# Logits of the second routing: from turned results instead of extra columns of w2

## What is computed

```python
x = attention(r, k, v, w, u)                       # [3072, 384]
# first mixture: top 1
logits = x @ w_gate + modality_bias[modality_id]
e_idx, gate = argmax(logits), softmax(logits)[e_idx]
for e in range(8):
    y[mask] = gate[mask] * (relu(x[mask] @ w1[e]) @ w2[e])
# second mixture: top 2 with noise
logits = y @ w_gate2
noise_scale = log1p(exp(y @ w_noise))
noisy = logits + noise_scale * noise
top2, weights = two largest of noisy, softmax over the two
out[mask] += weight * (relu(y[mask] @ w1b[e]) @ w2b[e])
```

## Time and profile before

| | us |
|---|---|
| three runs | 985.29, 985.99, 988.22 |
| median | 985.99 |
| the profiled execution | 981.03 |
| its span in the trace | 979.2 |

### The profile page before, as it was taken

One profiled execution on the slowest core, in us unless ns is written; L12 is line 12 of the kernel. 1 busy time (PEld: TensorE's weight loads), 2 busy tenths in 40 slices (PEclk: granted clock), 3 DMA queues, 4 the chain that ended last, 5 costly groups with the idle time before them and its releaser, 6 DMA issues.

```text
span 979.2 us, 22988 instructions
## 1 busy us (share of the span) xinstructions
PE 918.4 (94%) x7093; PEld 882.1 (90%) x7094; DVE 554.1 (57%) x1247; ACT 258.5 (26%) x493; POOL 423.3 (43%) x460
## 2 busy tenths in 40 slices
PE   5999999899889989999689999999999999999995
PEld 4888888899889989988689999999999999999995
DVE  8888989667754545648583544425335344443532
ACT  2222333124322323424220222203122231321210
POOL 7333333424655554446553343433434434344232
PEclk9999998989989999989899999999999999999998
DMA  8787899305411111123424534425333444513223
GB/s 266 229 263 256 268 353 359 111 3 188 169 34 51 33 34 41 42 98 93 139 66 90 131 96 115 111 44 117 104 52 101 121 104 112 112 32 54 45 48 51
DMA packets 61848, 115.96 MB, mean 118 GB/s; under 512 B 14352, under 2 KB 42192, under 8 KB 61776
## 3 DMA queue, kind: packets, MB, share of 16 engines
q1 hardware_dynamic: 39552, 75.37, 23.1%
q0 software_dynamic: 18336, 34.91, 17.2%
q10 hardware_dynamic: 3888, 4.80, 1.4%
HBM read 83.63 MB, written 31.51 MB: 118 GB/s over the span
## 4 chain that ended last, share of the span: by engine, by line
PE 78%; DVE 10%; issue 5%; POOL 2%; DMA 2%; DVEq 1%; ACT 1%; another core or an unknown queue 0%; ACTq 0%; SPq 0%; POOLq 0%
PE ps L1894 21%; PE ps L1895 20%; PE ps L1896 20%; PE ps L1841 3%; PE ps L1796 2%; PE ps L1800 2%; PE ps L1765 2%; PE ps L1742 2%; PE ps L1827 2%; PE ps L1854 1%; PE ps L1790 1%; DVE grow L1042 1%; PE ps L1750 1%; DVE hid_lo L1557 1%; DVEq L388 1%
## 5 line engine op out<-in xcount | busy, mean ns | idle before, releaser
L1894 PE MATMUL ps<-x_hi,weights 128*128 128x256 f32 x984 | 282.2, 287 | 18.9 <-issue 12.3
L1895 PE MATMUL ps<-x_lo,weights 128*128 128x256 f32 x984 | 281.2, 286 | 2.1 <-issue 2.0
L1896 PE MATMUL ps<-x_hi,weights 128*128 128x256 f32 x984 | 280.6, 285 | 2.5 <-issue 2.4
L1894 PE MATMUL ps<-weights,hid_hi 128*128 (+1 forms) x616 | 220.0, 357 | 3.4 <-DVE hid_lo L1557 2.3
L1895 PE MATMUL ps<-weights,hid_hi 128*128 (+1 forms) x616 | 212.5, 345 | 0.8 <-issue 0.8
L1896 PE MATMUL ps<-weights,hid_lo 128*128 (+1 forms) x616 | 211.5, 343 | 0.0
L1894 PEld LDWEIGHTS ps<-x_hi,weights 128*128 128x128 f32 x984 | 189.0, 192 | 21.0 <-issue 20.5
L929 ACT ACTIVATE hid_hi<-ps 128x512 fp32r<-128x512 f32 x164 | 97.1, 596 | 411.9 <-PE ps L1896 373.5
L1557 DVE SCALAR_TENSOR_TENSOR hid_lo<-ps,hid_hi 128x512 fp32r<-128x512 f32 x164 | 112.1, 690 | 153.2 <-ACT hid_hi L929 130.1
L1895 PEld LDWEIGHTS ps<-x_lo,weights 128*128 128x128 f32 x984 | 189.1, 192 | 6.3 <-issue 6.2
L1896 PEld LDWEIGHTS ps<-x_hi,weights 128*128 128x128 f32 x984 | 189.0, 192 | 2.9 <-issue 2.9
(11 more groups left out here) (313 smaller groups left out, 1148.8 us busy)
## 6 DMA issues: line engine op xcount, KB each, us to landing
stage<-in_w_dram SPq DMA_DIRECT2D x18, 1536.0 KB
kv_in<-in_kv_T_dram SPq DMA_DIRECT2D x24, 512.0 KB, 5.8
kv_in<-in_kv_T_dram SPq DMA_DIRECT2D x24, 448.0 KB, 4.0
w_in<-in_w_T_dram SPq DMA_DIRECT2D x24, 258.5 KB, 4.6
moe_rows<-zeros SPq DMA_DIRECT2D x26, 192.0 KB, 4.0
out_dram<-zeros SPq DMA_DIRECT2D x26, 192.0 KB
x_rows<-y_tok ACTq DMA_DIRECT2D x24, 192.0 KB
w2T_raw<-in_w_T_dram SPq DMA_DIRECT2D x2, 1536.0 KB
```

Source lines behind the costliest of these rows:

```text
L1894: pe.matmul(out_ps, hi, by_hi, start=first, stop=False)
L1895: pe.matmul(out_ps, hi, by_lo, start=False, stop=False)
L1896: return pe.matmul(out_ps, lo, by_hi, start=False, stop=final)
```

## The change

The 16 extra columns go. `CW` becomes 384, and `expert_columns`, `split_v`, `low_v`, `load_w2T` and the table `v_now` are removed with the transposed copy of w2. Instead, for every row, PE transposes the copied results (`turn_results`: six transposes of `sy`), ACT copies them out of PSUM (`turned_copies`, two), PE multiplies them with the 16 columns (`result_logits`: six products) and ACT copies the logits (`logits_copy`). The places in a step move: `turn_results` after `up` quarter 0, `result_logits` after quarter 1, `row_logits` after `hidden_low` 1, `row_first` after 2, `row_second` after 3, `row_ranks` just ahead of the last 12 products of `down`, and `row_places` behind both tiles of `split_x`. `turn_results` waits for `s_rankread`, which DVE raises in `row_places` when it has read the ranks of the row before, and for `s_oc[0]`, ACT's copy of the results. In step 0 of `l = 1`, `split_x` of both tiles now stands ahead of `second_order`.

```diff
-    CW = C + 2 * E
+    CW = C
...
+            def turned_copies(n, banks):
+                for t in range(TS):
+                    act.wait_ge(s_turn, n * TS + t + 1)
+                    act.nop(nofuse=True)
+                    act.activation(turned[t][:, :, :], banks[t], ACT.Copy).then_inc(s_turnc, 1)
+
+            def logits_copy(n, k):
+                act.wait_ge(s_logits, n)
+                act.nop(nofuse=True)
+                act.activation(raw_all[:, k, :, :], logit_ps, ACT.Copy).then_inc(s_raw, 1)
...
-                        act.activation(raw_all[:, u, t, :], o_ps[t][:, C:CW], ACT.Copy).then_inc(s_raw, 1)
-                        act.activation(sy[u][:, t, :], o_ps[t][:, 0:C], ACT.Copy).then_inc(s_oc[0], 1)
+                        act.activation(sy[u][:, t, :], o_ps[t], ACT.Copy).then_inc(s_oc[0], 1)
...
                 then(dve.tensor_tensor(row_pos[:, :, :], rank_ps, filled[:, 1:3, :], ALU.add))
+                dve.sem_inc(s_rankread, 1)
...
                     if peeled and s == 0:
                         hidden_low(0, 0)
+                        row_logits(last, raw_all[:, 0, :, :], last_nz, 2, last_dst)
+                        hidden_low(0, 1)
                         row_first(last, last_nz)
+                        hidden_low(0, 2)
                         row_second(last)
-                        hidden_low(0, 1)
-                        row_places(last, last_nz, 2, last_src, None)
-                        hidden_low(0, 2)
                         hidden_low(0, 3)
                         split_x(1, 1, 0)
+                        row_places(last, last_nz, 2, last_src, None)
+                        split_x(1, 1, 1)
                         second_order()
-                        split_x(1, 1, 1)
...
-                def expert_columns(n, v):
-                    pe.wait_ge(s_wT, n * 16 + 16)
-                    for m in range(FC):
+                def turn_results(n, rows, banks):
+                    pe.wait_ge(s_oc[0], 1 + n * TS)
+                    pe.nop(nofuse=True)
+                    for t in range(TS):
                         for c in range(CC):
-                            last = pe.matmul(v[:, m, :], w2T_raw[:, c, m * P:(m + 1) * P], gate_w[1][:, c, :],
+                            last = pe.transpose(banks[t][:, c, :], rows[:, t, c * P:(c + 1) * P], ident[:, :])
+                        last.then_inc(s_turn, 1)
+
+                def result_logits(n):
+                    pe.wait_ge(s_turnc, n * TS)
+                    pe.nop(nofuse=True)
+                    for t in range(TS):
+                        for c in range(CC):
+                            last = pe.matmul(logit_ps[:, t, :], turned[t][:, c, :], gate_w[1][:, c, :],
                                              start=(c == 0), stop=(c == CC - 1))
-                        last.then_inc(s_vmm, 1)
+                    last.then_inc(s_logits, 1)
...
                     up(s, 0, run)
+                    if l == 0 and (not peeled or s >= 2):
...
+                        turn_results(row, sy[0 if peeled and s == 2 else 1 - u], turn_ps)
                     up(s, 1, run)
+                    if row is not None:
+                        result_logits(row)
                     up(s, 2, run)
...
                     if l == 0 and peeled and s == 0:
                         pe.wait_ge(s_ytok, 1 + G)
-                        expert_columns(0, v0_ps)
...
-                        with pe.If(lookup(pe, v_now, s, 1) > 0):
-                            pe.wait_ge(s_hlo[0], s * 4 + 1)
-                            expert_columns((0 if early(s) else run) + 1, v_ps)
                     down_second(s, 0, run, two)
-                    if l == 0 and (not peeled or s >= 2 and s != 3):
-                        row_ranks(1 if peeled and s == 2 else s)
                     down(s, 0, run, 0)
                     slot_turn(l, s + 1, j + u, 1 - u, 1)
                     down_second(s, 1, run, two)
+                    if row is not None and not (peeled and s == 3):
+                        row_ranks(row)
                     down(s, 1, run, 0)
```

## The result

The changed kernel takes 989.77 us (median of 20 runs, 986.10 to 994.06), the kernel before 985.93 in 20 runs beside it (978.33 to 990.70). The ratio is 1.0052, with a 95% interval of 1.0034 to 1.0070: +3.8 us on the medians. The forecast was 987.9, in a range of 976 to 1000, with slower by over 0.3% as the likeliest of the three signs.

The account below looks back on a forecast made before the run. PE, busy 94% of the span, was taken as the bound. Terms of -5.7 us to the end of step 11, +5.9 at the turn and +1.7 for the clock gave +1.9 on 985.99, so 987.9, range 976 to 1000.

Parts of the forecast that it names:

- Step 0: Step 0 of l = 0: removing the 48 records of expert_columns and the slow clock behind them gives -8.9 us.
- rival D: Step 0: PE waits for DVE's counting of the first routing, half of 8.9 stays, about 992 us; chance 0.05.
- The price of a row: Each row: six transposes and six 16-column products cost 2.06 us, +1.74 a step with the narrower down.
- All three cost nothing as long as ACT and DVE are not held up: Each row: waits for ACT's result copies, ACT's transpose copies and s_rankread are covered, so they add nothing.
- rival C: Each loop step: new wait for row_any or copied transposes if 2.6 us slack is gone, about 998 us; chance 0.10.
- Steps 2 and 3: Steps 2 and 3 of l = 0: new row work less vanished waits, plus a wait for row_ranks(3), +2.9 us.
- Step 4: Step 4 of l = 0: loses its idle time and the slow clock behind it, 24.26 to 20.8 us, -3.5.
- Step 10: Step 10 of l = 0: -10.1 us for removed records and slow clock, +3.5 for new work and waiting, -6.6 together.
- The turn: Step 12 and l = 0 to l = 1: PE's wait moves to down of step 1 and grows, +5.9 us.
- Rival B: Turn to l = 1: not paid, +5.9 becomes about -1 us, total about 979 us; chance 0.28.
- The clock: Loop steps: one more stretch of 3.41 us at clock 0.50 than before, +1.7 us.
- Rival A: Logits to end of up: clock falls in most loop steps, +12 us, total about 1000 us; chance 0.17.

Follow-up runs that it names:

- e4: Changed kernel with the old 16 extra columns of w2 made again, unused, in steps 0 and 10: 978.81 us, ratio 1.0229 to the kernel before.
- e6: The kernel before, unedited, traced on one of the experiments' chips: 955.85 us, ratio 0.999.
- e5: The changed kernel, unedited, on one of the experiments' chips: 965.41 us, ratio 1.0095 to the kernel before.
- e3: Changed kernel with each row's six transposes and six 16-column products made twice: 999.62 us, ratio 1.0427 to the kernel before.
- e8: e7 plus e1's bank, row_second right behind row_first, and in slot 2 ACT's result copies ahead of soft_noise(2): 952.57 us, ratio 0.9956 to the kernel before.
- e1: Changed kernel with a separate PSUM bank for the turned x of the second tile: 960.9 us, ratio 1.0034 to the kernel before.
- e2: Changed kernel with the last row's results, logits and choice ahead of the gathered rows and split_x at the turn: 964.08 us, ratio 1.0067 to the kernel before.
- e7: Second form of e2, gathered rows turned first and split_x of slot 0 first in DVE's queue: 962.27 us, ratio 1.0047 to the kernel before.
- e11: Changed kernel with row_second right behind row_first in DVE's queue, bank still shared: 964.75 us, ratio 1.0078 to the kernel before.
- e12: Changed kernel with two dummy ACT activations ahead of hid_hi of quarter 1 in the loop steps and behind them: 964.52 us, ratio 1.0074 to the kernel before.
- e10: Changed kernel with each row's six transposes made four times over, products once: 988.84 us, ratio 1.0321 to the kernel before.

## Where the prediction was right and where it was wrong

**Step 0** (-8.9): -10.8 in the first pair of traces, -10.6 in the second, and e4 gives 10.8 for what was removed. Right in kind, 2 us too small, and rival D falls.

**The price of a row** (2.06 us, +1.74 a step): right. e6 and e5 give +1.70, e3 gives 1.99 for the row. The 12 records take 1.26 us in a loop step of the changed kernel, not 1.46. On the first chip the steps grew by 1.2 only, because of a term that the sum left out: the 1.1 us of gaps in `up` were taken as part of the kernel in both sums, and they went. The five steps cost +5.0 there instead of +8.7, and 1.8 of the difference is step 8, which got its clock back (below).

**"All three cost nothing as long as ACT and DVE are not held up"**: the condition failed on the first chip. The 2.6 us of slack that rival C counted for row_any were the wrong slack. `row_first`, done ahead of `hidden_low` 0 in the kernel before, now stands between `hidden_low` 2 and 3 and so just ahead of `split_x` of the first tile, and PE asks for that x_lo before it asks for row_any; 13.1 us of such waits in steps 3 to 11 of the first trace of the changed kernel, 3.39 and 3.81 of them in steps 10 and 11. So rival C's mechanism was there, with another place, and paid for by the gaps that went.

**Steps 2 and 3** (+2.9): +7.0 in both pairs. The named waits for x did go, but the step gained a wait of 2.03 us for ACT's copies of slot 2's results, which stood behind `soft_noise(2)`, and 1.66 us of "issue" at the loop's entry, right behind a wait for row_any. The first was in ACT's queue and I had not walked it; e8 takes it out. That one the sum had put at nothing.

**Step 4** (-3.5): +1.8 in the first pair, -0.8 in the second. The slow clock did not go with the idle time: in e5 step 4 is 100% busy and takes 21.30 us at a clock of 0.92, behind the idle stretch at the end of step 3. In e1, e2, e7, e11 and e12 it takes 19.9 at 1.00, so this clock comes and goes from run to run.

**Step 10** (-6.6): -4.2 and -2.2. The term -10.1 for the 48 records was mis-sized: it took all their time and the slow clock behind them as gained. e4 shows 2.6 us for them: without them PE waits for the row's choice, which `low_w1` has cut in pieces, and a clock of 0.91 follows all the same.

**The turn** (+5.9): right in place and kind, and in size where it can be read. From the start of step 12 to step 2 of `l = 1` it is +5.9 between e6 and e5, +8.2 in the first pair. The exact 5.9 is luck in part: 1.6 of it falls in step 12, which the sum put at 0, and 4.3 behind it. `second_order` starts 17.7 us after `up` of step 0 in e5 against 14.3 in e6 (475.63 - 457.90, 469.78 - 455.44). e2 took the cause away and steps 0 and 1 shrank by 8.9 us. Rival B falls.

**The clock** (+1.7): no loop step of 5 to 9 fell below 1.00 after the change, and step 8, at 0.92 before, recovered. So this term was rather -1.7. Over the whole trace the granted clock went from 0.968 to 0.974. Rival A falls for one row's work; e3 shows that its mechanism is real at twice the work.

The sum of +1.9 came near the measured +3.8 through errors of both signs and with luck: too little for steps 2 to 4 and 10, too much for step 0, the loop steps and the clock. It was worked out on the profiled execution, and there the change costs 9.0 us; on the other chip the medians are 8.7 apart, which the forecast's own range of 983.5 to 992.5 would not have held.

## What to carry to other kernels

When work moves from a few large blocks into every step, look for what stood idle around the blocks: part of their price may come back as a wait for an engine whose queue they covered (here 48 records were worth 2.6 us in step 10 and 10.8 in step 0). When a chain is put into a queue in pieces, check every consumer of what now stands behind the pieces, the earliest first, and mend a shared buffer and the order together, since either alone only moves the wait. And a difference of 0.5% can hinge on the series of measurements: the same pair gave 1.0052 in one and 1.0095 in another, on another chip.

## What the chips showed that I had not expected

The kernel before takes 985.9 us in the first series and 956.7 to 957.6 on the three chips of the experiments. In the traces (23.1 us apart) the difference lies in steps 4 to 12 of `l = 0`: 20.35 against 18.10 us for the same loop step, while a step of `l = 1` takes 17.63 and 17.64. On the first chip PE has gaps marked "issue" in `up` there, and ACT starts a `hid_hi` late with "remote" as the releaser (in step 6 quarter 0 by 4.0 us in the kernel before, quarter 1 by 2.7 in the changed one), in the same stretch of each step, while POOL issues its small transfers. In the trace of before, instruction transfers fall in step 5 (three of them) and in none of steps 6 to 8, while the gaps are in all four, so they are not simply that. I did not find the cause.

Narrow FP32 products, 16 columns wide, hold PE at 100% busy, and behind 24 records of them the clock fell in three of five loop steps (0.71 over the 5.93 us that follow, e3); behind 24 transposes of 128 columns in FP32 it did not in any (e10).

POOL's subtraction of 3.5 us held DVE up in the tables of `l = 1` in both kernels: in the changed one a one-operand DVE instruction on 8 elements, from 504.43, lasted 4.15 us beside it (POOL from 505.01), in the one before a comparison of 304 elements lasted 4.37 us instead of the 0.47 of the same one ahead of it.
